# A gated-memory attention kernel on Trainium2: gate chain rearranged, the second chunk's logs spread by transfers, masked halves and zero rows left out of the loads

## The reference, cut to what matters

```python
# 1: gated memory, token by token, per batch and head
m_new = max(f_gate[t] + m, i_gate[t])
f_stab = exp(f_gate[t] + m - m_new);  i_stab = exp(i_gate[t] - m_new)
C = f_stab * C + i_stab * outer(v[t], k[t]);  n = f_stab * n + i_stab * k[t]
y[t] = sigmoid(o_gate[t]) * (C @ q[t]) / max(abs(n . q[t]), 1)
# 2: x is y with the heads side by side, (2, 768, 320)
h = relu(x @ w_in)                      # 320 -> 1024, halves u and v
v_n = (v - mean(v)) / sqrt(var(v) + 1e-6)
x2 = (u * (w_spatial @ v_n + b_spatial)) @ w_out
# 3
h2 = relu(x2 @ w_in2)                   # 320 -> 1024
c = conv_w[0] * h2[t-1] + conv_w[1] * h2[t] + conv_w[2] * h2[t+1]
out = (h2 * sigmoid(c)) @ w_out2
```

## Time and profile before

| | |
|---|---|
| median of 3 runs | 283.63 us |
| profiled execution | 282.72 us, its span 280.8 us |
| TensorE busy | 271.8 us, 97% |
| VectorE busy | 201.1 us, 72% |
| ScalarE busy | 160.0 us, 57% |
| GpSimd busy | 65.5 us, 23% |
| DMA | 25.47 MB |

### The profile page before, as it was taken

The page is one execution under the profiler, slowest core; times in us unless marked ns, Lnnn a source line. Parts: engine busy times, 40 slices in busy tenths (PEclk is TensorE's granted clock), DMA queues, the critical chain, the costliest instruction groups (busy, mean ns, idle before and its releaser), DMA issues.

```text
span 280.8 us, 5262 instructions
## 1 busy us (share of the span) xinstructions
PE 271.8 (97%) x1981; PEld 260.5 (93%) x1981; DVE 201.1 (72%) x368; ACT 160.0 (57%) x320; POOL 65.5 (23%) x98
## 2 busy tenths in 40 slices
PE   7999999999999999999999999999899999899995
PEld 6898899889999999999999989999899999899995
DVE  3686987787988987755467784455867766866694
ACT  3848776996886764414244112256665667666763
POOL 2281831166464222072000880000000000000000
PEclk9999999999999999999999999999999999999999
DMA  6999975465646000009300000000000000300004
GB/s 168 270 277 338 333 225 196 145 213 184 201 145 215 2 0 2 0 7 297 110 2 0 0 0 2 0 0 2 0 4 0 0 0 2 138 2 4 0 0 142
DMA packets 12284, 25.47 MB, mean 91 GB/s; under 512 B 1595, under 2 KB 7259, under 8 KB 12259
## 3 DMA queue, kind: packets, MB, share of 16 engines
q1 hardware_dynamic: 11683, 24.48, 28.0%
q10 hardware_dynamic: 576, 0.66, 0.7%
HBM read 23.11 MB, written 2.02 MB: 89 GB/s over the span
## 4 chain that ended last, share of the span: by engine, by line
PE 84%; DVE 7%; ACT 4%; issue 3%; ACTq 0%; POOL 0%; DVEq 0%; POOLq 0%
PE bank L556 18%; PE bank L613 13%; PE bank L598 13%; PE bank L581 8%; PE bank L542 7%; PE bank L524 7%; PE bank L503 6%; PE bank L473 4%; PE bank L481 2%; PE bank L435 2%; PE bank L509 1%; PE bank L456 1%; PE bank L492 1%; DVE decay L914 1%; DVE convd L1076 1%
## 5 line engine op out<-in xcount | busy, mean ns | idle before, releaser
L556 PE MATMUL bank<-wsp_hi,vn_hi 128*128 128x384 f32 x96 | 32.2, 335 | 0.0
L556 PE MATMUL bank<-wsp_hi,vn_lo 128*128 128x384 f32 x96 | 32.1, 334 | 0.0
L556 PE MATMUL bank<-wsp_lo,vn_hi 128*128 128x384 f32 x96 | 32.1, 334 | 0.0
L613 PE MATMUL bank<-wo_hi,hg_hi 128*128 128x320 f32 x96 | 29.9, 312 | 1.8 <-DVE hg_lo L1089 0.9
L748 ACT ACTIVATE gt_hi<-gated_t 128x384 fp32r<-128x384 f32 x16 | 8.4, 525 | 37.5 <-DVE gated_t L1039 37.5
L613 PE MATMUL bank<-wo_lo,hg_hi 128*128 128x320 f32 x96 | 29.6, 309 | 0.0
L613 PE MATMUL bank<-wo_hi,hg_lo 128*128 128x320 f32 x96 | 29.6, 308 | 0.0
L1072 DVE SCALAR_TENSOR_TENSOR tap<-h,conv_w,tap 128x768 f32<-128x768 f32 (+1 forms) x17 | 16.5, 969 | 16.6 <-ACT tap L780 16.6
L703 ACT ACTIVATE decay<-log_in,cols 128x128 f32<-128x128 f32 x80 | 25.5, 391 | 3.8 <-PE bank L503 3.8
L503 PEld LDWEIGHTS bank<-v_aug,decay 128*128 128x128 f32 x192 | 24.1, 191 | 2.4 <-DVE decay L914 1.3
L503 PE MATMUL bank<-v_aug,decay 128*128 128x42 f32 x192 | 24.4, 277 | 0.6 <-DVE decay L914 0.4
(11 more groups left out here) (164 smaller groups left out, 762.5 us busy)
## 6 DMA issues: line engine op xcount, KB each, us to landing
log_in<-neg_m SPq DMA_DIRECT2D x10, 512.0 KB, 4.8
qk<-qk SPq DMA_DIRECT2D x18, 160.0 KB
wsp_raw<-w_sp SPq DMA_DIRECT2D x6, 384.0 KB, 4.1
win_raw<-w_in SPq DMA_DIRECT2D x4, 512.0 KB, 6.3
v_aug<-v SPq DMA_DIRECT2D x12, 168.0 KB, 5.1
og_b<-og SPq DMA_DIRECT2D x4, 480.0 KB, 8.9
kw<-k SPq DMA_DIRECT2D x10, 160.0 KB, 5.8
wo_raw<-w_out SPq DMA_DIRECT2D x8, 160.0 KB, 2.9
```

Of the source, the lines that this page charges most:

```text
L556: op = pe.matmul(p_mix[m % 2][:, 0:NB], vs[:, b * NC + c, ds_], ws[:, c, ts], start=(i == 0), stop=(i == len(terms) - 1))
L613: op = pe.matmul(p_y[c][:, 0:HD], g[t % 2][:, cs], w[:, t, :], start=(t == 0 and i == 0), stop=(t == KF - 1 and i == 2))
```

## The change

1. `i` is loaded on ScalarE's queue. TensorE reads the end of `b` as soon as it is there, VectorE copies it into `reset` then, and scans the ends of `A` from PSUM; `m_prev` is transposed without waiting for `m_last`, which has a bank of its own. The filler of the gate chain goes from 7, 3 and 2 to 4, 1 and 1 (`keep_warm`), that of chunks 0 and 1 from 3 to none.
2. `EARLY` is 1: chunk 1's logs come through DRAM too. `neg_m` has two halves of 64 tokens; a chunk's first half is loaded to 64 partitions only, its second to 128, as two transfers. The rest is filled once with -1e30 by GpSimd. `weigh(0, 1)` stands before the copies of `cols` and `dec`.
3. q and k come in 40-row pieces for every chunk; the rows between are cleared once, on VectorE for buffer 0 and GpSimd for the others.
4. `win5` is loaded once (64 rows); ScalarE copies the rounded half up, GpSimd subtracts (`narrow_low`), and clears `win5_lo` at the start. The `v` half of `w_in` is loaded after the stores and loads of the logs of chunk 1, the `og` piece 3:6 after the loads of chunk 3.
5. The first sigmoid stands behind the exponents of chunk 0.
6. In layer 3, `high(0)` stands before `relu(1)`; `write_y(0)` behind `sigmoid(9)` on ScalarE and before `gated(9)` on VectorE; SP issues all stores of batch 0.

```diff
-EARLY = 2
+EARLY = 1
+HL = L // 2
-    log_in = [a.put(f"log_in{p}", [128, H, L], F32) for p in range(RING)]
+    log_in = [a.put(f"log_in{p}", [128, 2, H, HL], F32) for p in range(RING)]
-    p_ends, p_prev, p_warm = p_t[0:1, 0:2 * R], banks[0][0:R, 0:2], banks[3]
+    p_ends, p_ends_a, p_warm = p_t[0:1, 0:R], banks[5][0:1, 0:R], banks[3]
+    p_prev, p_last = banks[0][0:R, 0:1], banks[2][0:R, 0:1]
...
@@ sync_program
-        sp.dma_start(sc["i"][:, :], ig).then_inc(sem("ld_gates"), 16)
...
-            for ps in [slice(0, KS)] if n < RING else [rows(0), rows(1)]:
+            if n < RING:
+                sp.wait_ge(sem(f"pad{n}"), 1)
+            for ps in (rows(0), rows(1)):
...
+            for half in range(2):
+                ps = slice(0, HL if half == 0 else 128)
+                sp.dma_start(log_in[n % RING][ps, half, :, :].rearrange("p h t -> p (h t)"),
+                             neg_m[half, n:n + 1, :].to_broadcast([ps.stop, H * HL])).then_inc(sem(f"ld_log{n % RING}"), 16)
...
-        sp.dma_start(og_b0[:, 0:3, :], og[:, 0:3, :]).then_inc(sem("ld_o0"), 16)
         load_qk(0)
         load_k(0)
         load_v(0)
-        load_in(v_half, "v")
+        sp.dma_start(og_b0[:, 0:3, :], og[:, 0:3, :]).then_inc(sem("ld_o0"), 16)
         sp.wait_ge(sem("neg_ready"), 1)
+        for half in range(2):
+            sp.dma_start(neg_m[half, :, :].rearrange("n (h t) -> (n h) t", h=H), sc["negM"][:, half * HL:(half + 1) * HL]
+                         ).then_inc(sem("neg_kept"), 16)
         load_qk(1)
+        sp.wait_ge(sem("neg_kept"), 32)
+        load_log(1)
         load_k(1)
         load_v(1)
-        sp.wait_ge(sem("neg_kept"), 16)
+        load_in(v_half, "v")
         load_log(2)
...
-        sp.dma_start(og_b0[:, 3:6, :], og[:, 3:6, :]).then_inc(sem("ld_o0b"), 16)
         load_log(RING)
         load_k(state_chunk(KRING))
         load_qk(RING)
         load_v(RING)
+        sp.dma_start(og_b0[:, 3:6, :], og[:, 3:6, :]).then_inc(sem("ld_o0b"), 16)
@@ gpsimd_program
+        pool.wait_ge(sem("state_zero"), 2)
+        for p in range(1, RING):
+            pool.memset(qk_in[p][32:64, :, :, :], 0.0).then_inc(sem(f"pad{p}"), 1)
+        for p in range(RING):
+            pool.memset(log_in[p][HL:128, 0, :, :], NEG).then_inc(sem("log_pad"), 1)
+        pool.memset(win5_lo[LO:128, :].bitcast(F32), 0.0).then_inc(sem("win_ready"), 1)
...
         weigh_k(0)
+        mask_log(1)
         weigh_k(1)
-        clear_low(0, v_half)
-        mask_first(1, 0)
-        mask_log(2)
-        mask_first(1, 1)
         decay_state(1)
+        narrow_low(0, v_half)
+        mask_log(2)
         weigh_k(2)
@@ tensor_program
-        keep_warm(7)
-        pe.wait_ge(sem("scan_done"), 3)
+        keep_warm(4)
+        pe.wait_ge(sem("scan_done"), 1)
+        pe.matmul(turned(p_ends[:, 0:R]), sc["b"][:, L - 1:L], by_chain, start=True, stop=True).then_inc(sem("ends_ready"), 1)
+        pe.wait_ge(sem("scan_done"), 3)
+        pe.matmul(turned(p_ends_a), sc["A"][:, L - 1:L], by_chain, start=True, stop=True).then_inc(sem("ends_ready"), 1)
...
+        pe.wait_ge(sem("chain_done"), 2)
+        pe.transpose(p_prev, m_prev[0:1, :, :].rearrange("p n h -> p (n h)"), one[:, :]).then_inc(sem("prev_ready"), 1)
         pe.wait_ge(sem("chain_done"), 3)
+        pe.transpose(p_last, m_last[0:1, :, :].rearrange("p n h -> p (n h)"), one[:, :]).then_inc(sem("last_ready"), 1)
+        keep_warm(1)
...
-        keep_warm(1)
         in_chunk(0, 0)
-        first_logs(1, 0)
         in_chunk(0, 1)
         to_state(0)
-        first_logs(1, 1)
...
-                keep_warm(2, p_t)
@@ scalar_program
+        act.dma_start(sc["i"][:, :], ig).then_inc(sem("ld_igate"), 16)
         act.wait_ge(sem("gate_const"), 5)
-        act.activation(warm[0:R, 0:1], ones_r[:, 0:1], ACT.Sigmoid)
-        open_gates(0)
-        act.activation(warm[0:R, 1:2], ones_r[:, 0:1], ACT.Exp)
+        act.activation(warm[0:R, 0:1], ones_r[:, 0:1], ACT.Exp)
...
         exp_log(0, 0)
         exp_log(0, 1)
-        win_high("v", v_half)
+        open_gates(0)
         exp_log(1, 0)
+        narrow_high("v", v_half)
         for n in range(1, NS):
+            if n == 1:
+                xt_high(0)
+                win_high("v", v_half)
...
         x2_high(1, 1, 2)
+        high(0)
         relu(1)
-        high(0)
...
+            if e < UNITS - 2:
+                sigmoid(e)
             if e == UNITS // 2 + 1:
                 write_y(0)
-            if e < UNITS - 2:
-                sigmoid(e)
@@ vector_program
+        dve.memset(qk_in[0][32:64, :, :, :], 0.0).then_inc(sem("pad0"), 1)
...
-        dve.tensor_copy(flat(ends_a), p_t[0:1, R:2 * R])
...
         weigh(0, 0)
+        weigh(0, 1)
...
-        weigh(0, 1)
-        first_low(0, v_half)
         for n in range(1, NS):
...
             if n == 1:
+                first_low(0, v_half)
                 new_state(n)
...
+            if e == UNITS // 2 + 1:
+                write_y(0)
             if e < UNITS - 2:
                 gated(e)
-            if e == UNITS // 2 + 1:
-                write_y(0)
```

More of the change, by code:

```diff
@@ L144, in build_program @@
     one = s.put("gate_one", [1, 1], F32)
-    ends_a, reset, m_end = (s.put("gate_" + n, [1, H, B, NC], F32) for n in ("enda", "reset", "mend"))
+    reset, m_end = (s.put("gate_" + n, [1, H, B, NC], F32) for n in ("reset", "mend"))
     m_prev, m_last = (s.put("gate_" + n, [1, NS, H], F32) for n in ("mprev", "mlast"))
@@ L320, in sync_program @@
         for b in range(B):
-            for c in (1, 2, 3, 5):
+            for c in range(NC) if b < B - 1 else (1, 2, 3, 5):
                 sp.wait_ge(sem("y_dve" if c % 2 else "y_act"), b * 3 + c // 2 + 1)
@@ L374, in spatial_low, with narrow_low @@
                                ).then_inc(sem("wsp_ready"), 1)
-        def clear_low(i, cs):
-            pool.wait_ge(sem("win_hi"), 2 * i + 2)
-            pool.memset(win5_lo[LO:128, cs].bitcast(F32), 0.0).then_inc(sem("win_ready"), 1)
+        def narrow_low(i, cs):
+            pool.wait_ge(sem("win_hi"), 3 * i + 1)
+            pool.tensor_tensor(win5_lo[0:K5, cs], win5_raw[0:K5, cs], win5_hi[0:K5, cs].bitcast(F32), ALU.subtract
+                               ).then_inc(sem("win5_low"), 1)
         mask_first(0, 0)
@@ L799, in write_y, with narrow_high @@
                 act.activation(y[:, c, :], p_y[c][:, 0:HD], ACT.Copy).then_inc(sem("y_act"), 1)
-                if c != 2:
+                if b == B - 1 and c != 2:
                     act.wait_ge(sem("y_act"), b * 3 + c // 2 + 1)
                     act.dma_start(out[b, c * L:(c + 1) * L, :], y[:, c, :]).then_inc(sem("stored"), 16)
+        def narrow_high(half, cs):
+            act.wait_ge(sem(f"ld_win5{half}"), 16)
+            act.activation(win5_hi[0:K5, cs], win5_raw[0:K5, cs], ACT.Copy).then_inc(sem("win_hi"), 1)
         def win_high(half, cs):
@@ L818, in scalar_program @@
             if n == 2:
+                narrow_high("u", u_half)
                 win_high("u", u_half)
@@ L822, in scalar_program @@
                     spatial_high(n - spatial_step(0), blk)
-            if n != LATE + 1:
+            if n not in (1, LATE + 1):
                 xt_high(n - 1)
@@ L939, in vector_program @@
         dve.wait_ge(sem("prev_ready"), 1)
-        link(dve.tensor_copy(prev_col[:, :], p_prev[:, 0:1]))
+        link(dve.tensor_copy(prev_col[:, :], p_prev))
         dve.tensor_scalar(sc["negM"][:, :], sc["A"][:, :], prev_col[:, 0:1], -1.0, ALU.max, ALU.mult
                           ).then_inc(sem("neg_ready"), 1)
+        dve.wait_ge(sem("a_raw"), 1)
+        dve.tensor_copy(cols[:, 2, :], p_cols[:, 2, 0:R]).then_inc(sem("cols_ready"), 1)
         dve.wait_ge(sem("neg_ready"), 1)
```

85 lines of the change are left out of this document (38 added, 47 removed).

## The result

| | before | after |
|---|---|---|
| median | 283.61 us (4 runs, 283.47 to 284.72) | 287.39 us (4 runs, 286.55 to 288.54) |
| ratio | | 1.0128, 95% interval 1.0079 to 1.0176 |
| span of the profiled execution | 280.8 us | 285.1 us |
| third transposes of x start | 34.87 us | 40.85 us |
| first spatial product starts | 109.60 us | 115.41 us |

The time is above the range and on the wrong side of no change. (Some executions of one kernel, before's too, run for a time at a lower granted clock and are several us longer; the medians here count them, the ratios leave them out.) The last two rows say where it went. I use "the third transposes of x" (`transpose_x(2)`, right behind the end of x(2)) as a milestone throughout.

What follows compares the result with a forecast made beforehand. It took TensorE, at full clock and almost always busy from 35 us on, as the bound. Gains of 1.5 at 35 us plus 0.8 and 0.85 near the end, 3.15, say 3.2, gave 280.4 us; range 278.9 to 282.3.

Steps and rivals of the forecast that it cites:

- the wait for the weights: TensorE before the first hidden_v: a new wait of 1.5 to 2 us.
- 3 us of work: TensorE up to chunk 1: dropped log matmuls (2.05) and filler (0.71 and a little) save 3 us of work.
- rival D: TensorE's faster level may come later with less filler; logs and scores up to 1.7 more: 281.3 us, chance 0.07.
- 4.7 us, covered: GpSimd's nine clearing units at the start take 4.7 us, 2.7 to 7.4, with 1 us of cover left.
- 1.14 us given back to VectorE: VectorE before x(2): the win5 subtraction's move to GpSimd gives back 1.14 us.
- Gate chain: Start of the kernel, scans to negM: negM ends at 5.7 instead of 7.83, 2.1 us sooner.
- Up to chunk 1: Chunk 1's logs through DRAM: negM store lands at 9.3, log pieces at 13.0, exponents out at 15.6.
- The weights: Later weight loads: v half lands at 16.6, hidden_v(0) starts at 19.0, og lands at 28.4; gain at 35 us 1.5.
- Rival A: Early loads land late, win and og eat the early gain: early gain 0.3, 281.7 us, chance 0.16.
- Rivals B and C: Early loads: B at 338 GB/s, 279.3 us, chance 0.11; C at 189 GB/s, 286.9 us, chance 0.04.
- Near the end: From 190 us on: moving high(0) gains 0.8 us, earlier copies of y gain 0.85.
- Rival E: An end reordering moves its stall elsewhere, one gain gone: 281.3 us, chance 0.06.

Runs made afterwards that it cites:

- e10_refill: The changed kernel with all filler calls of the kernel before put back, memsets unmoved: 287.97 us, ratio 1.0081.
- e6_mimic: The changed kernel with memsets moved off the blocked copy, before's filler, and eight filler calls where chunk 1's log matmuls stood: 288.66 us, ratio 1.0047.
- e13_gate_filler: The kernel before with only the gate chain's filler cut, from 7, 3 and 2 calls to 4, 1 and 1: 293.65 us, ratio 1.0399.
- e1_nolock: The changed kernel with GpSimd's memsets moved behind the gate chain and the first masks, filler still lean: 286.15 us, ratio 1.0126.
- e14_slim: e7_gate_end plus the slimmer loads, with GpSimd instead of VectorE subtracting win5: median 290.07 us.
- e7_gate_end: The kernel before with the new gate chain, the first sigmoid's new place and the end reorderings, all of before's filler kept: 284.46 us, ratio 0.9944.
- e4_end: The kernel before with the end reorderings (part 6) alone: 282.33 us, ratio 0.9942.
- e15_seven: The kernel before with only the first filler cut, from 7 calls to 4: 291.43 us (284.04 to 298.31), no ratio.
- e9_order: e7_gate_end with the change's order of loads, chunk 1's logs staying in TensorE: 287.97 us, ratio 1.0145.
- e18_slim_filled: e14_slim with 8 instead of 2 filler calls ahead of the first transposes of x: 283.92 us, ratio 1.0031.
- e17_order_filled: e9_order with 12 instead of 2 filler calls ahead of the first transposes of x: 283.06 us, ratio 0.9992.
- e11_v_first: e6_mimic with the v half of w_in loaded ahead of the negM store again: 285.99 us, ratio 1.0082.
- e2_filler: The changed kernel with five more keep_warm calls behind the m_prev transpose, memsets unmoved: 284.55 to 290.71 us, ratio 1.0106.
- e8_fill_gaps: e6_mimic with 4 filler calls first instead of 7, and 3 behind the m_prev transpose: 287.52 us, no ratio.
- e5_lean: The kernel before with all the change's filler cuts and nothing else of it: 294.59 us, ratio 1.0315.

## Why the prediction was wrong

**The sum of the loss.** At the milestone +5.98 us, where 1.5 less than before was forecast. The profiled executions of e10_refill and e6_mimic, with the level kept until past 20 us, have +3.0: so about 3 us go to the filler, and 3 to the wait for the weights with its own fall of the level (1.90, and 3.5 us at half rate). The blocked copy adds nothing that shows: e10_refill has it and e6_mimic doesn't, and both stand at 37.9. This split rests on one execution of each. The end gives 1.5 back. 5.98 - 1.5 = 4.5, measured 4.3.

**The step that failed: the clock.** The forecast's own sum had no term for TensorE's level. It booked the dropped log matmuls and filler as "3 us of work" saved and the new wait for the weights at its own 1.5 to 2 us, as if both left the level at 2.4 GHz. Measured, TensorE ran at the 1.2 GHz level for 20.5 us from 8.7 on. The level stood in rival D alone: "logs and scores take up to 1.7 more, much of it under the wait for `win`", a chance of 0.07. I had the cause, had read from the earlier trace rows that the first filler ran at the lower level, and costed only those 16 + 16 matmuls, as if the level rose by 9 us regardless. It didn't rise for 20: 10 us in e13_gate_filler, about 3 in the change itself. Even the 32 alone cost more, 2.55 in e1_nolock (3.68 for 2.05 and 2.08 for 1.16). The mechanism was a rival, its size was wrong by a factor of 2 to 6, and with it the sign of the result. The signal that I had named for it, log matmuls at half rate after 5.7, is the one that e1_nolock shows. The wait behind which the level fell once more, 1.90 in e10_refill, had the length that I forecast; what it does to the level stood in no rival.

**GpSimd's memsets.** "4.7 us, covered". Their length was right (2.78 to 7.00 for the nine units, 4.2), the cover was counted on GpSimd alone. I didn't ask who else is stopped while they run. The Trainium skill, "SBUF — State Buffer", section "Who interferes with whom", says that VectorE's copies in their two-port modes and GpSimd's instructions take one pair of ports as an exclusive lock, and that the later one waits fully. The trace agrees: 1.89 us against 0.22 with the memsets moved. The copy, begun at 5.18, was let in between none of the memsets, which followed each other until 7.00. The same section of the Trainium skill says that a `tensor_tensor` with both inputs in SBUF contends with GpSimd's reads; the 2.10 us against 1.22 in e14_slim agree. I had booked the `win5` subtraction, moved to GpSimd, as 1.14 us given back to VectorE. After, on VectorE and GpSimd:

```profile
21.78 2.27 DVE L1125 TENSOR_TENSOR win_lo<-win_raw,win_hi 128x1024 fp32r<-128x1024 f32 x1 [0.22 <-ACT win_hi L823]
```

```profile
20.60 1.27 POOL L394 TENSOR_TENSOR win_lo<-win_raw,win_hi 64x512 fp32r<-64x512 f32 x1
21.82 1.14 POOL L378 TENSOR_SCALAR_AFFINE_SELECT log_in<-log_in 128x1024 f32<-128x1024 f32 x1
22.94 1.70 POOL L361 TENSOR_TENSOR kw<-kw,cols 128x320 f32<-128x320 f32 x1
```

The subtraction left on VectorE takes 2.27 us: 1.2 until GpSimd's mask ends at 22.96, then its own 1.1, during which GpSimd's next operation takes 1.70 instead of 0.74. Nearly all of the 1.14 is lost again.

**Gate chain.** `negM` ends at 7.41, not 5.7; at 6.15 without the memsets. Without the block the date was right to 0.45. But seven calls of filler were not slack to be cut: they set both the chain's pace and the clock. What the chain gains by their going, the clock takes (e1_nolock), and with them in place it gains 0.55 of the 2.1 (e7_gate_end).

**Up to chunk 1.** The `negM` store landed by 9.35 (forecast 9.3), and that was luck: it left at 7.43 instead of 5.9 and took 1.9 us instead of 3.4. The log pieces landed at 15.9 (13.0) and 3.8 to 6.0 us after their issue, though the queue was almost empty: a share of 0.36 and 80 GB/s from 8 to 10 us, in the first of the stretches after. I had dated them from bytes at 290 GB/s. That step was 2.9 us off; why a small load takes so long there stays open.

**The weights.** The `v` half landed near 19.2 (16.6), `hidden_v(0)` started at 24.30 (19.0). TensorE had no wait of its own there; with the level kept until then it has one, 1.07 in e6_mimic and 1.90 in e10_refill. Rival A had these landings, at 0.16, with 281.7: without the clock, it too was too cheap. (It puts 648 KB of other loads before `og`; by my own sums, 4536 less 3024 less the 480 of `og`, they are 1032 KiB.) `og` landed at 31.3, not 28.4. Rivals B and C (early loads at 338, late at 189 GB/s through `og`) didn't happen; `og`'s sigmoid at 33.56 waited for nothing. That the slimmer loads bring anything is not shown by any run.

**Near the end.** Both terms were right: 1.65 forecast, 1.5 in the change, 1.4 to 1.6 in e4_end, waits as forecast (0.3 left where I had 0.1). Rival E is out.

What stays open: how the 6 us divide in the change's usual executions; how much the slimmer loads would give with VectorE's subtractions undisturbed; and why single executions of the same kernel, e15_seven and e7_gate_end above all, now keep the level and now lose it.

## What to carry to other kernels

Read TensorE's level from the length of one kind of matmul in each stretch, at the start above all, and treat every filler call as load-bearing until a run without it says otherwise. Price a new wait of TensorE not at its length but at its length plus what the level may cost behind it (here 3.0 us of wait made 6 to 7), and try filler in its place before giving up an edit; then look at ten runs, not at one profile, since one kernel loses the level in some executions and not in others. Before work goes to GpSimd "under cover", list VectorE's copies and two-input operations in the same microseconds: they pay for it.

## What the runs showed of the hardware

- A gap of 1.56 or 3.0 us in TensorE's work was followed by 20 and 10 us at the 1.2 GHz level, and the same place filled with matmuls was not (e14_slim, e9_order; e18_slim_filled, e17_order_filled). Gaps of 1.90 and 2.49 us were followed by 3.5 us of it (e10_refill, e11_v_first), and it also came with no gap above 0.6 us close before it (e2_filler, e8_fill_gaps, e18_slim_filled). No run here shows what decides.
- At the lower level a busy share of 27.49 in 28 us went with over 20 us at the lower level (e13_gate_filler). With six more filler calls the log matmuls at 7.89 already ran at 0.13 each.
- The granted clock on the page reads 1.00 for the start of kernels whose matmuls there take twice their time (e1_nolock, e5_lean, e13_gate_filler).
- Back-to-back memsets of GpSimd held off a 96-element copy of VectorE until the last of them was done: 1.89 us for 0.22 of work. A `tensor_tensor` of VectorE with both inputs in SBUF took 2.10 and 2.27 us for 1.22 beside GpSimd's reads (e14_slim, after).
